# Attention ahead of two expert layers: other steps for side work, and list rows scattered one tile per step

## The reference

```
attention: 4 batches, 8 heads, 576 queries, head size 64
  k_p, v_p = means of k, v over 8 neighbouring rows      # 72 keys per batch and head
  attn = softmax(q @ k_p^T / 8); x = attn @ v_p           # x: 2304 tokens x 512
moe: logits = x @ w_gate + log1p(exp(x @ w_noise)) * noise      # 8 experts
  top 2 experts per token, softmax weights over the two
  out = sum over the two of weight * relu(x @ w1[e]) @ w2[e]    # hidden size 1024
moe2: p = probs / sum(probs); out = sum over 4 experts of p[:, e] * relu(x @ w1b[e]) @ w2b[e]
```

## Time and profile before

| | |
|---|---|
| Median of 3 runs | 1427.7 us (1425.74 to 1430.73) |
| Profiled execution, its own time | 1431.1 us |
| Its span, first to last instruction | 1429.4 us |
| TensorE busy | 1358.5 us, 95% of the span |
| VectorE, ScalarE, GpSimd busy | 701.0, 394.2, 692.4 us |
| Mean granted TensorE clock | 0.977 of 2.4 GHz |
| DMA moved | 133.71 MB, mean 94 GB/s |

### The profile page before, as it was taken

One profiled execution on the slowest core, in us unless ns is written; L12 is line 12 of the kernel. 1 busy time (PEld: TensorE's weight loads), 2 busy tenths in 40 slices (PEclk: granted clock), 3 DMA queues, 4 the chain that ended last, 5 costly groups with the idle time before them and its releaser, 6 DMA issues.

```text
span 1429.4 us, 22020 instructions
## 1 busy us (share of the span) xinstructions
PE 1358.5 (95%) x6985; PEld 1195.6 (84%) x6986; DVE 701.0 (49%) x1292; ACT 394.2 (28%) x736; POOL 692.4 (48%) x464
## 2 busy tenths in 40 slices
PE   6885699999999999998999999999999999999997
PEld 5875588888888888887888898889889989989986
DVE  5658322222222122314876686765655555555564
ACT  2443122222222212423343343422322222232210
POOL 2225288482744729297867686442233222233202
PEclk9978799999999999999999999999999999999999
DMA  9837243342424324412422332210001000000002
GB/s 275 285 107 287 96 134 103 129 132 73 161 73 132 97 101 153 143 53 68 133 74 74 104 105 72 82 67 30 30 29 59 29 29 29 29 29 29 15 0 89
DMA packets 63604, 133.71 MB, mean 94 GB/s; under 512 B 5496, under 2 KB 23048, under 8 KB 63448
## 3 DMA queue, kind: packets, MB, share of 16 engines
q1 hardware_dynamic: 43320, 84.69, 18.1%
q0 software_dynamic: 8272, 26.49, 5.7%
q10 hardware_dynamic: 11952, 21.76, 4.7%
HBM read 108.22 MB, written 30.74 MB: 97 GB/s over the span
## 4 chain that ended last, share of the span: by engine, by line
PE 50%; DVE 2%; issue 1%; ACT 0%; DVEq 0%; ACTq 0%
PE banks L1022 26%; PE banks L995 23%; DVE hD L1806 1%; DVE acc L1849 0%; PE banks L981 0%; DVE block_sums L1823 0%; ACT hD L1334 0%; DVE acc L1852 0%; DVE block_sums L1829 0%; DVE x_ops L1802 0%; ACT acc L1224 0%; DVE block_sums L1820 0%; DVE x_sums L1783 0%; ACT unit_w L1356 0%; DVE block_sums L1817 0%
## 5 line engine op out<-in xcount | busy, mean ns | idle before, releaser
L1022 PE MATMUL banks<-unit_w,hD 128*128 128x512 f32 x1728 | 404.6, 391 | 3.3 <-DVE acc L1849 2.6
L1022 PEld LDWEIGHTS banks<-unit_w,hD 128*128 128x128 f32 x1728 | 322.3, 188 | 72.9 <-DVE acc L1849 7.1
L995 PE MATMUL banks<-x_ops,unit_w_hi 128*128 128x384 f32 x1344 | 342.4, 335 | 6.0 <-issue 2.6
L995 PEld LDWEIGHTS banks<-x_ops,unit_w_hi 128*128 128x128 f32 x1344 | 243.3, 188 | 11.5 <-issue 5.4
L1849 DVE SCALAR_TENSOR_TENSOR acc<-banks,sorted_record,acc 128x512 f32<-128x512 f32 x270 | 200.5, 748 | 104.4 <-PE banks L1022 100.9
L875 PE MATMUL banks<-expert_w,xT 128*128 (+1 forms) x960 | 232.7, 398 | 1.5 <-DVE xT L1585 1.5
L901 PE MATMUL banks<-expert_w,hT 128*128 (+1 forms) x960 | 226.2, 392 | 2.7 <-issue 2.7
L530 POOL TENSOR_TENSOR unit_w_lo<-raw_weights,unit_w_hi 128x512 fp32r<-128x512 f32 (+1 forms) x60 | 63.0, 1071 | 339.5 <-ACT unit_w_hi L1350 339.5
L995 PE MATMUL banks<-x_ops,unit_w_lo 128*128 128x384 f32 x672 | 225.1, 335 | 0.0
L901 PEld LDWEIGHTS banks<-expert_w,hT 128*128 128x128 f32 x960 | 181.1, 189 | 40.6 <-issue 3.0
L875 PEld LDWEIGHTS banks<-expert_w,xT 128*128 128x128 f32 x960 | 180.0, 191 | 38.9 <-issue 2.1
(11 more groups left out here) (232 smaller groups left out, 1292.5 us busy)
## 6 DMA issues: line engine op xcount, KB each, us to landing
raw_weights<-in_w SPq DMA_DIRECT2D x32, 1024.0 KB
raw_weights<-in_w1b SPq DMA_DIRECT2D x32, 512.0 KB
raw_weights<-in_w2b SPq DMA_DIRECT2D x32, 512.0 KB, 3.3
x_rows<-x_sorted ACTq DMA_DIRECT2D x43, 256.0 KB, 2.7
y_sorted<-y_rows ACTq DMA_DIRECT2D x40, 256.0 KB
qT<-in_q SPq DMA_DIRECT2D x3, 1152.0 KB, 16.1
kv_half<-in_k SPq DMA_DIRECT2D x5, 576.0 KB, 10.9
kv_half<-in_v SPq DMA_DIRECT2D x5, 576.0 KB, 10.7
```

The costliest lines, as they stand in the source:

```text
L995: mm = pe.matmul(dst[:, 0:HALF], (w1h, w1l)[st][par][:, b, c, :], x2o[blk][:, a, mv, c, :], start=(first and t == 0), stop=(t == 5), skip_ ...
L1022: mm = pe.matmul(bank[5 + t % 3][:, :], hD[:, buf, st, c, P * t:P * t + P], w2o[par][:, mv, D * c:D * c + D], start=(n == 0), stop=(n == 3 ...
```

## The change

Side work moves to other steps in the five tables. SyncE's order changes in two places. `scatter` waits before each tile until the values of a given later tile have been multiplied. ScalarE copies the logits ahead of the value block, and `LOW_AT` may name several halves for one step.

```diff
-        K_AT, V_AT = {2: 1, 6: 2, 8: 3}, {4: 1, 7: 2, 9: 3}
-        V_BLOCKS_AT = {0: 0, 4: 1, 8: 2, 11: 3}
-        HIGH_AT = {9: 0, 10: 1, 15: 2, 18: 3}
-        LOW_AT = {11: (0, 0), 12: (0, 1), 13: (1, 0), 15: (1, 1), 16: (2, 0), 17: (2, 1)}
+        K_AT, V_AT = {2: 1, 5: 2, 9: 3}, {4: 1, 8: 2, 12: 3}
+        V_BLOCKS_AT = {0: 0, 4: 1, 9: 2, 13: 3}
+        HIGH_AT = {11: 0, 14: 1, 17: 2, 19: 3}
+        LOW_AT = {13: ((0, 0), (0, 1)), 15: ((1, 0),), 16: ((1, 1),), 18: ((2, 0),), 19: ((2, 1),)}
@@ SyncE
             kv_load(1, 0)
             q_load(0, first=Q_FIRST)
+            kv_load(1, 1)
             q_load(1)
-            kv_load(1, 1)
...
             kv_load(3, 0)
-            load_raw(0, 0, 0, None)
             kv_load(3, 1)
             q_load(3)
+            load_raw(0, 0, 0, None)
             load_raw(1, 0, 1, None)
@@ GpSimd, scatter(g)
                 pool.wait_ge(pos_ok, g + 1)
-                for t in range(*GROUPS[g]):
+                first, end = GROUPS[g]
+                for t in range(first, end):
+
+                    pool.wait_ge(x_ps, min(end + 3 + t - first, NT))
                     for kk in range(2):
@@ ScalarE
                 if s + 1 < NT:
                     exps(s + 1)
+                if s >= 2:
+                    logit_copy(s - 2)
                 if s in V_BLOCKS_AT:
                     v_block(V_BLOCKS_AT[s])
-                if s >= 2:
-                    logit_copy(s - 2)
@@ VectorE
-                if s in LOW_AT:
-                    low_half(*LOW_AT[s])
+                for r, half in LOW_AT.get(s, ()):
+                    low_half(r, half)
```

## The result

The changed kernel takes 1413.0 us (median of 8 runs, 1411.1 to 1418.4); the kernel before took 1425.9 us beside it (8 runs, 1420.8 to 1430.7). The ratio is 0.9904, with a 95% interval of 0.9884 to 0.9924. In a second set the ratio was 0.9885 (0.9856 to 0.9915), at 1412.3 us against 1426.8. The forecast of 1412.8 us was met in the median; three of the eight runs took 1416.4 to 1418.4 us. Its terms were not all met, and what they missed was made up by differences between executions.

What follows compares the result with a forecast made beforehand. TensorE is busy without a break behind 155 us, so only an earlier start of the experts' first product counts, through attention-stage waits and the DMA-bound changeover. -3.0 - 3.1 - 14.6 + 0.7 + 1.7 = -18.3 from 1431.1: 1412.8 us, range 1406 to 1430.

Steps and rivals of the forecast that it cites:

- Scatter waits: Attention stage, GpSimd: one tile's scatters per step instead of trains of eight removes late signals; -14.6 us, bounds 0 to -15.8.
- the four slow steps go: Steps 10, 11, 13 and 14 fall to 4.32 us each, 15.84 us less before 1.2 us of real work is deducted.
- Logit copy: Step 5: ScalarE's copy ahead of the value block ends TensorE's wait; -3.0 us, bounds 0 to -4.1.
- Poolings: Steps 7 and 8: pooling moved to step 5 covers VectorE's late subtraction; -3.1 us, bounds 0 to -3.4.
- SyncE's order: Early loads of values, queries and first weight piece reordered: 0 us, bounds -1 to +2 if step 3 met late queries.
- VectorE's loaded steps: Steps 13 to 15: weight parts moved later load VectorE; +0.7 us, from 0 to 2.44 plus a clock loss of 1.7.
- Loads later: Changeover: fourth weight piece and fills asked for 3.6 us later delay the scatters' landing; +1.7 us, bounds -0.6 to +3.6.
- three scatters draining ahead of the load: Changeover: some three scatters drain in the gap before the fourth piece's load, saving 1.9 us.
- spread loss: Rival: every scatter pair delays signals, steps 7 to 14 all slow; +20.3 us there, +7.0 in all, 1438 us; chance 0.12.
- the first list load: Sign of being right, at the changeover: ScalarE's first load of list rows still about 20 to 23 us behind the last values.
- rival of unrelated signals: Rival, attention stage: late signals have nothing to do with scatter trains; -3.7 us, 1427.4 us; chance 0.16.
- half-stays rival: Rival, attention stage: one of two pairs of late signals stays (7 us), so 1420 us; chance 0.22.
- the prediction's second rival: Rival, attention stage: late signals unrelated to scatter trains, only the other moves count; -3.7 us, 1427.4 us; chance 0.16.

Runs made afterwards that it cites:

- changed, again: A second profiled execution of the unedited changed kernel, on another chip: 1411.5 us, span 1409.8 us.
- e1: Kernel before plus only the tile waits (each tile's two scatters wait for a later tile's values): 1419.1 us, ratio 0.9933 to the kernel before.
- e2: Changed kernel without the tile waits, so a group's scatters go out in one train: 1427.8 us, ratio 0.9994 to the kernel before.
- e11: Changed kernel without the tile waits, run again on another chip: 1429.1 us, ratio 0.9997 to the kernel before.
- e5: Changed kernel with the wait only at every second tile of a group, meant as trains of four scatter issues: 1413.6 us, ratio 0.9970.
- e6: Changed kernel with ScalarE's value block ahead of the logit copy again: 1415.5 us, ratio 0.9986 to the kernel before.
- e10: Kernel before, unedited, run and profiled once more: 1426.1 us, span 1424.4 us.
- e7: Changed kernel with the old steps of poolings and value blocks: 1417.4 us, ratio 0.9997 to the kernel before.
- e3: Changed kernel with SyncE's old order of queries, values and first weight piece: 1412.8 us, ratio 0.9879 to the kernel before.
- e4: Changed kernel with the second expert's first two weight pieces and the y_sorted fills waiting until list rows have landed: 1407.5 us, ratio 0.9840.
- e9: Changed kernel, unedited, measured again in another set: 1412.3 us, ratio 0.9885 to the kernel before.
- e8: Changed kernel with the old steps of the weight parts: 1412.5 us, ratio 0.9964 to the kernel before.
- e12: Changed kernel with late fills and second-expert pieces, SyncE's old early order, and VectorE's last two low halves later: 1404.7 us, ratio 0.9835.

## Why the prediction was right, step by step

Worked out from the first profile of before to changed, again (spans 1429.4 and 1409.8, 19.6 us apart):

- **Scatter waits: forecast -14.6, measured -12.7.** This is the six steps from the transposition of the exponentials in step 9 to that in step 15, 42.9 us before and 30.2 after (31.3, or -11.6, in the first profile of the changed kernel). The cause is shown by e1, e2 and e11. What fell short is "the four slow steps go": late signals of up to 1.5 us stayed. In e5, where none stayed, these steps take 28.4 us, which is the forecast's 28.3. In changed, again, step 9 is 1.3 and step 13 0.5 us longer than there. In step 9 the train was not broken up at once, since the first three tiles' waits were already fulfilled or nearly so when the group's positions came, and six issues went out from 55.35 to 64.07 with a gap of 1.14 us. ScalarE then waited 2.08 us for the transposed exponentials. In that execution TensorE ran on past step 9 at full clock, as the 1.23 us rows show; in the first profile of the changed kernel it did not. The second half of step 14's value products, put at 1.2 us, took 1.3.
- **Logit copy: forecast -3.0, measured -3.25** (9.58 to 6.33 us). The undone edit e6 brought the same 2.18 us wait back, but cost 1.9 us: half of the term was the slow value products of one execution. In e10 the kernel before took 8.0 us for step 5.
- **Poolings: forecast -3.1, measured -3.3**; undone together with the later poolings and value blocks (e7) 3.8 us.
- **SyncE's order: forecast 0.** Right for the median (e3). In the first profile of the changed kernel step 3 took 9.53 us against 6.59 before, 2.9 us more, which is beyond the upper bound of +2.
- **VectorE's loaded steps: forecast +0.7, measured 0.** Steps 13 to 15 run 4.8, 5.6 and 4.4 us, and step 13 runs 4.3 us in five of the other profiles with these weight steps. In changed, again, TensorE waits for no subtraction in these steps.
- **Loads later: forecast +1.7, measured +2.9.** From the last values' products to the first list rows before 152.00 - 122.37 = 29.6 us, after 134.53 - 102.01 = 32.5. This term of the sum was undersized, and the part of it that rests on three scatters draining ahead of the load failed; the full shift of 3.6 us is nearer. The table below bears it out: 29.6 to 30.9 us in the profiles with the old weight steps, 32.3 to 34.0 with the new ones and the fills where they were. By the Trainium skill (DMA: Bandwidth & Descriptors, Queues, rings and completion order) an engine alternates by packet, as the 5 packets against 5 in the earlier trace rows agree; the sum that the prediction set beside that rule, 1.9 us worse than its own, was the better one for this term. e4 shows the place: with the fills and the second expert's pieces gone from it, the last scatter lands in 3.1 us.
- **Not in the forecast, -2.9:** 0.8 us ahead of step 5, where only SyncE's order differs, and 2.1 us behind the first list rows, by which 1277.4 us became 1275.3. Behind them nothing was changed; the same stretch took 1277.3 us in the second profile of the kernel before and between 1274.8 and 1278.2 in the other profiles, e4's 1283.5 aside, so this is the variation between executions.

The sum of the measured terms is -12.7 - 3.25 - 3.3 + 2.9 - 2.9 = -19.25, against -18.3 forecast. That the total came out so near is partly luck. The two largest errors, +1.9 and +1.2, have the same sign, and what made up for them is mostly variation (-2.9). The pair of executions matters as well: against the first profile of the changed kernel the span shrank by 12.7 us, and the medians are 12.9 and 14.5 us apart in the two sets, where the forecast meant 14.9 from its median.

**Two errors of the prediction that did not touch its sum.** The price of the spread loss is wrong: steps 7 to 14 already took 107.94 - 52.99 = 54.95 us before, and eight steps of 6.86 are 54.88. So that rival adds nothing there, instead of 5.7, and its time is near 1432 us, not 1438. And the first list load stood 149.18 - 122.37 = 26.8 us behind the start of the last values before the change, not 20 to 23; after it, 27.7 and 29.9.

The rival of unrelated signals fell by e1 and e2. The spread loss did not come: most steps with pairs run at full clock, though step 10 of the changed kernel's first profile did not, behind the late signal of step 9. The half-stays rival fell by the profile, since no long late signal stayed.

What no rival had: the parts do not add. The waits alone give 9.6 us, the other moves alone (e2, e11) nothing, both together 13 to 15. The stretches of the profiles show most of it. In us; steps 5 to 8 and 9 to 14 are taken from transposition to transposition of the exponentials, the changeover from the start of the last values' products to the first list rows on TensorE:

| Profile | Steps 5 to 8 | Steps 9 to 14 | Changeover |
|---|---|---|---|
| before | 25.96 | 42.89 | 29.63 |
| before again (e10) | 23.65 | 40.45 | 30.10 |
| waits alone (e1) | 25.27 | 29.66 | 30.53 |
| other moves alone (e2) | 19.40 | 43.15 | 32.33 |
| other moves alone (e11) | 19.40 | 44.54 | 33.69 |
| changed | 19.41 | 31.34 | 32.54 |
| changed, again (e9) | 19.42 | 30.15 | 32.52 |
| changed, SyncE's old order (e3) | 19.40 | 28.97 | 34.02 |
| changed, trains of four (e5) | 19.41 | 28.38 | 33.27 |
| changed, old weight steps (e8) | 19.41 | 32.16 | 30.92 |

The other moves win 4.2 to 6.6 us in steps 5 to 8. They give back 2 to 4 in the changeover, and without the waits up to 4 more in steps 9 to 14, which took longer in e2 and e11 than in either profile of the kernel before. Why these steps took longer is open.

**Open also:** what makes a signal late when scatters are dense. Shown is that the long delays come with unbroken trains of eight issues and go when the train is broken up, not through what path, nor whether the number of scatters in flight or their bytes per time decide. And why the kernel before took 1418 us on one chip, with the same trains in its code. Had that chip no late signals, only the other moves would be left, for which the prediction's second rival has 3.7 us; e5 measured 4.3. No profile of the kernel before on that chip shows it.

## What to carry to other kernels

A wait labelled "remote", on two engines at once and beside a train of software DMAs, is worth an experiment on its own: spacing the issues by a wait on work that happens anyway costs one line and gave 9.6 us by itself, some two thirds of this change's gain in the two sets where the kernel before was slow. Price an idle gap of TensorE with the slow steps behind it, which cost here half as much again (2.5 us behind a stall of 5.3). A wait on work that is already done spaces nothing: look at when each wait is fulfilled. And before moving work ahead of a stage that ends in scatters, count the bytes that are queued there: fills and weight pieces that nobody needs yet were worth 5 us once they stood behind the scatters (e4 against e3).

## What the runs showed of the hardware

Signals from TensorE reached both ScalarE and VectorE late, with up to 4.8 us of idle time there, while TensorE's own instructions went on until they needed the answer. The long delays stand in steps 9 to 14 of every profile with trains of eight (before, e2, e10, e11), the first of e10's being the shortest, at 1.82 us of idle time. With pairs of issues the nine profiles (both of the changed kernel, e1, e3, e4, e6, e7, e8, e12) show no lag over 1.5 us in steps 5 to 17, and e1, e6, e7 and e8 none over 0.3. Two HBM-to-HBM fills (15 tiles of 256 KB in all) hold back the software queue: in 124 to 126 us of the kernel before it moved 0.01 MB while the third train of scatters was in it.
